# A fused attention, Fourier and MLP kernel: GpSimd's decay work waits for VectorE's progress, and decayed keys get two buffers

## What is computed

```python
for b in range(nb):                       # blocks of a sequence
    intra = einsum('bhic,bhjc->bhij', qb, kb) * Dmask     # scores, masked with the decay
    intra = einsum('bhij,bhjd->bhid', intra, vb)
    inter = einsum('bhid,bhde->bhie', qb * lam_pow, kv_state)   # decayed queries
    out[block] = intra + inter
    kb_dec = kb * rev_pow                                       # decayed keys
    kv_state = lam_block * kv_state + einsum('bhsd,bhse->bhde', kb_dec, vb)
# then, with x of 2 x 768 x 512:
u  = x + real(fft(fft(x, axis=seq), axis=hidden))
un = layernorm(u)
x2 = u + relu(un @ w_ch1) @ w_ch2                         # 512 -> 2048 -> 512
out = (sigmoid(causal_conv5(x2)) * (x2 @ w_val)) @ w_out
```

## Time and profile before

| | us |
|---|---|
| median of 3 runs | 451.03 |
| lowest and highest | 449.82 to 452.81 |
| the profiled execution | 451.31 |
| its span | 449.5 |

### The profile page before, as it was taken

The page is one execution under the profiler, slowest core; times in us unless marked ns, Lnnn a source line. Parts: engine busy times, 40 slices in busy tenths (PEclk is TensorE's granted clock), DMA queues, the critical chain, the costliest instruction groups (busy, mean ns, idle before and its releaser), DMA issues.

```text
span 449.5 us, 7168 instructions
## 1 busy us (share of the span) xinstructions
PE 434.8 (97%) x2934; PEld 415.0 (92%) x2934; DVE 264.5 (59%) x433; ACT 150.2 (33%) x284; POOL 146.4 (33%) x97
## 2 busy tenths in 40 slices
PE   9799869899999999999999999999999999999997
PEld 8688769789999999999999999999999999889985
DVE  2446897978356944454424327948557548999220
ACT  1145342274212331113342227353124233515221
POOL 1334461158422222523539223234224251500000
PEclk9899989999999999999999999999999999999999
DMA  6968720224022030202112212012112110001112
GB/s 202 382 211 273 206 79 2 65 59 158 2 93 94 0 95 1 93 1 94 55 41 95 54 41 93 29 66 95 34 61 93 32 63 2 1 1 70 71 47 93
DMA packets 13889, 36.52 MB, mean 81 GB/s; under 512 B 1561, under 2 KB 3105, under 8 KB 13857
## 3 DMA queue, kind: packets, MB, share of 16 engines
q1 hardware_dynamic: 13856, 36.07, 24.0%
HBM read 32.91 MB, written 3.15 MB: 80 GB/s over the span
## 4 chain that ended last, share of the span: by engine, by line
PE 85%; DVE 9%; DMA 2%; issue 2%; ACT 1%; SPq 1%; DVEq 0%
PE ps L532 10%; PE ps L534 10%; PE ps L555 10%; PE ps L533 10%; PE ps L554 10%; PE ps L553 10%; PE ps L644 2%; PE ps L643 2%; PE ps L642 2%; PE ps L621 2%; PE ps L622 2%; PE ps L623 2%; PE ps L406 2%; PE ps L489 2%; DMA chunks<-in_qkv 2%
## 5 line engine op out<-in xcount | busy, mean ns | idle before, releaser
L728 ACT ACTIVATE hh<-ps 128x384 fp32r<-128x384 f32 x64 | 31.5, 493 | 176.8 <-PE ps L534 176.8
L992 DVE SCALAR_TENSOR_TENSOR hl<-ps,hh 128x384 fp32r<-128x384 f32 x64 | 35.3, 556 | 87.0 <-ACT hh L728 87.0
L532 PE MATMUL ps<-cen_h,w1h_a 128*128 128x384 f32 x128 | 43.9, 343 | 0.5 <-DVE hl L992 0.5
L532 PE MATMUL ps<-cen_h,w1h_b 128*128 128x384 f32 x128 | 44.2, 345 | 0.0
L534 PE MATMUL ps<-cen_h,w1l_b 128*128 128x384 f32 x128 | 43.1, 337 | 0.0
L555 PE MATMUL ps<-hh,w2l_b 128*128 128x384 f32 x128 | 43.1, 337 | 0.0
L533 PE MATMUL ps<-cen_l,w1h_a 128*128 128x384 f32 x128 | 43.1, 337 | 0.0
L534 PE MATMUL ps<-cen_h,w1l_a 128*128 128x384 f32 x128 | 43.1, 337 | 0.0
L554 PE MATMUL ps<-hl,w2h_b 128*128 128x384 f32 x128 | 43.1, 337 | 0.0
L553 PE MATMUL ps<-hh,w2h_b 128*128 128x384 f32 x128 | 43.1, 337 | 0.0
L533 PE MATMUL ps<-cen_l,w1h_b 128*128 128x384 f32 x128 | 43.0, 336 | 0.0
(11 more groups left out here) (161 smaller groups left out, 1016.9 us busy)
## 6 DMA issues: line engine op xcount, KB each, us to landing
raw_a<-in_mlp SPq DMA_DIRECT2D x16, 512.0 KB, 4.7
raw_b<-in_mlp SPq DMA_DIRECT2D x16, 512.0 KB, 4.4
chunks<-in_qkv SPq DMA_DIRECT2D x12, 512.0 KB, 5.5
chunks<-in_qkv SPq DMA_DIRECT2D x22, 256.0 KB, 5.7
out<-out_sb SPq DMA_DIRECT2D x12, 256.0 KB, 2.0
raw_a<-in_val SPq DMA_DIRECT2D x2, 512.0 KB, 4.4
raw_b<-in_out SPq DMA_DIRECT2D x2, 512.0 KB, 4.4
seq_c<-const_seq SPq DMA_DIRECT2D x1, 768.0 KB, 6.0
```

Source lines behind the costliest of these rows:

```text
L532: mm(bank, wh_, xh, start=r == 0, stop=False)
L728: nc.scalar.activation(hh[:, slot, j], ps[j][:, 0:TB], ACT.Relu).then_inc(s_hh, 1)
L992: stt(hl[:, slot, j], ps[j][:, 0:TB], 0.0, hh[:, slot, j].bitcast(F32), ALU.max, ALU.subtract).then_inc(s_hl, 1)
```

## The change

GpSimd gets a wait at the head of each chunk from n = 6 on, on a count that VectorE raises (`turn_of`), and `kd` gets a second buffer, so that kd(n) waits for the state product two chunks back instead of the last. For n = 6 and 7 the wait is for the end of radix4(n - 2), for n = 8 for two_even, for n = 9 for chunk_pair(0, 2), for n = 10 for third_pair, and for n = 11 for add_pair(0, 1).

```diff
-            kd = sb_in(att, "kd", [P, H, Dh])
+            kd = sb_in(att, "kd", [P, 2, H, Dh])
...
-                        m = mm(ps[KV][par * Dh:(par + 1) * Dh, hp * Dh:(hp + 1) * Dh], kd[:, 2 * hp + par, :],
+                        m = mm(ps[KV][par * Dh:(par + 1) * Dh, hp * Dh:(hp + 1) * Dh], kd[:, kds(n) % 2, 2 * hp + par, :],
...
-                if kds(n) >= 2:
-                    pool.wait_ge(s_kv, kds(n) - 1)
-                tt(kd[:, :, :], kr[c], decay[:, :, 0:1].broadcast_to([P, H, Dh]), ALU.mult).then_inc(s_kd, 1)
+                if kds(n) >= 3:
+                    pool.wait_ge(s_kv, kds(n) - 2)
+                tt(kd[:, kds(n) % 2], kr[c], decay[:, :, 0:1].broadcast_to([P, H, Dh]), ALU.mult).then_inc(s_kd, 1)
...
+            def turn_of(n):
+                if n in (NC, NC + 1):
+                    pool.wait_ge(s_r4, R4 * (n - 1))
+                elif n == NC + 2:
+                    pool.wait_ge(s_r6, 6)
+                elif n == NC + 3:
+                    pool.wait_ge(s_r6, 10)
+                elif n == NC + 4:
+                    pool.wait_ge(s_r6, R6)
+                elif n == NC + 5:
+                    pool.wait_ge(s_u, added_u(0, 1))
+
             decay_keys(0)
             for n in range(1, N):
+                turn_of(n)
                 if n % NC < NC - 1:
                     decay_keys(n)
```

## The result

| | before | changed |
|---|---|---|
| median, us (runs) | 451.03 (6) | 446.87 (6) |
| lowest and highest | 449.82 to 452.81 | 445.40 to 448.07 |
| the profiled execution | 451.31 | 448.07 |
| its span | 449.5 | 446.3 |

The ratio of the two medians is 0.9908. Estimated from all the runs of both it is 0.9893, with a 95% interval of 0.9865 to 0.9921: between 0.8 and 1.35% faster. The forecast for the median was 447.1.

A forecast was written before the change was run, and what follows sets the result against it. VectorE and GpSimd were taken to block each other in SBUF, with TensorE waiting before a full MLP. The path, 69.16 - 65.3 = 3.9 us shorter, took 451.31 to 447.4, 447.1 for the median; range 445.6 to 449.0.

The forecast's parts named there:

- Chunk 7: kd(7) waits for radix4(5), so L898 takes 0.28 instead of 1.15: minus 0.87 us, in full on the path.
- L914 absorbed by mask(8)'s wait: In two_even, L914 waits 0.8 us for qd(7); VectorE's 1.12 us idle before mask(8) hides it, leaving 0.3.
- Chunk 8: kd(8) runs after two_even; L919's start to L920's end goes from 2.39 to 1.60 us: minus 0.79.
- Chunk 9: qd(9) still collides with L925, whose length goes from 1.16 to 1.42 us: plus 0.26.
- Chunk 10: kd(10), qd(10) and qd(11) leave the last three sums; L928 to L930 go from 4.89 to 2.04 us: minus 2.85.
- Behind it: After L930, radix4(6) waits for qd(10) and loses 0.8 us; seq_pair(0, 1) starts at 65.3 instead of 69.16.
- The front, zero: Early chunks: qd(3) delays radix4(1) but is hidden, and kd(4)'s keys land too late to collide; cost zero, bounds 0 and 0.8.
- The rule held against the change: A skill rule has the blocked engine start 0.25 us later in three collisions: gain an estimated 0.5 less, 3.4.
- queries slip through: Rival, chance 0.20: qd(10) doesn't go ahead of radix4(6), and qd(8), qd(9) collide less; gain 4.9, 446.1 us.
- the gates do little: Rival, chance 0.08: VectorE waits for TensorE's scores at every mask, only the first 0.87 us reaches the end; 450.2 us.
- The front collision: Rival, chance 0.17: kd(4)'s keys land before 25.8 us, so kd(4) meets radix4(1); gain 3.1, 447.9 us.
- The clock falls: Rival, chance 0.05: TensorE's clock falls in the gap from 63.7 to 65.3 us and stays low to 78; net 2 slower, 453.

The follow-up runs named there:

- e2: The changed kernel without its second key buffer, so the gates alone; 446.42 us, ratio 0.9915 to before.
- e3: The kernel with one key buffer and all gates, cut to only the gates of chunks 10 and 11; 447.90 us, ratio 0.9942 to before.
- e6: The changed kernel with one gate more, qd(10) waiting for radix4(6); 446.47 us, ratio 0.9892 to before.
- e5: The changed kernel with qd(8), qd(9) and qd(10) computed for only 8 of 128 tokens; 443.94 us, ratio 0.984 to before.
- e10: The changed kernel with one gate more, hidden_sum(0, 2) on GpSimd waiting for radix4(8); 445.84 us, ratio 0.9877 to before.
- e8: The changed kernel with the first MLP weights loaded after chunk 4 instead of chunk 3, so chunk 4's keys land earlier; 447.78 us, ratio 0.9919 to before.
- e1: The changed kernel without its gates, so two key buffers alone; 451.03 us, ratio 1.0011 to before.
- e7: The changed kernel with batch 0's decayed keys waiting for the last state product, as before the change; 446.76 us, ratio 0.9904 to before.
- e9: The kernel before with 13 unused products on TensorE in the wait before seq_pair(0, 0), to keep the clock up; 449.62 us, ratio 0.9978 to before.

## Why the prediction was right

The forecast was 447.1 us, with 3.9 us of gain on the path; measured were 446.87 us, and 4.27 to seq_pair(0, 1). The forecast gave 0.69 to a change within 1% and 0.27 to a faster one; with 0.8 to 1.35% the result lies on the border of the two, or just beyond. Times of the changed profile are given less 1.21 us here, on the common point.

- *Chunk 7*, minus 0.87: L898 0.28, and TensorE's wait fell by 0.86.
- *L914 absorbed by mask(8)'s wait*: 0.3 was to be left of 1.12; 0.43 was. mask(8) at 50.25, forecast 50.29.
- *Chunk 8*, minus 0.79: L919's start to L920's end 1.47 instead of 1.60; before 2.39. e2 shows that the second buffer is what buys it.
- *Chunk 9*, L925 1.42: 1.38.
- *Chunk 10*, minus 2.85: exactly; L930 ended at 60.32, forecast 60.50. e3 shows this gate, with that of chunk 11, at 2.7 of 4.3, its cost in radix4(6) included.
- *Behind it*: radix4(6) lost 0.69, forecast 0.8; e6 takes it away. seq_pair(0, 1) started 4.27 earlier, forecast 3.9. I put the 0.37 down to small sizes: I charged 0.1 for each gate's handover, which took 0.08, and let an operation start at the recorded end of the one before, where it starts 0.08 before that. Behind seq_pair(0, 1), where I had the same chain, another 0.23 was gained to the MLP (4.50 in all); hidden_sum(0, 1) met radix4(7)'s L892 for 0.2 (0.3 forecast).
- *The front, zero*: it held, in this profile by a margin of nothing. All engines in order of time around radix4(1) of the changed kernel:

```profile
26.92 0.28 DVE L898 TENSOR_TENSOR zin<-esum 128x128 f32<-128x128 f32 x1
...
27.23 1.06 POOL L1156 TENSOR_TENSOR kd<-chunks,decay 128x512 f32<-128x512 f32 x1 [1.05 <-DMA chunks<-in_qkv]
...
27.50 0.71 PE L464 MATMUL ps<-hid_c,zin 128*128 128x128 f32 x4
```

radix4(1) ends at 27.20, 0.3 before TensorE needs it, and kd(4), whose keys came late, starts 0.03 behind. On the common point these are 25.99 (25.98 forecast) and 26.02 (26.2). In the three other profiles with this front and the same loads kd(4) starts later behind radix4(1): 0.3 us in e5, 1.7 in e6, 1.4 in e10. e8 shows the price when the keys don't come late. In how many executions of the changed kernel that happens stays open.

- *The rule held against the change* from the Trainium skill, SBUF — State Buffer, section "A bandwidth-pool intuition that's wrong", was an estimated 3.4. The measured 4.27 speaks for the rows: L914, L919 and L925 ended 0.54 to 0.55 after the qd that held them and are 0.68 long, so it began before the blocker's recorded end, here as before.
- *The rivals*: "queries slip through" is what e5 builds, and it was not the case; "the gates do little" fell with L930. "The front collision" is what e8 builds; it cost 0.7. "The clock falls" was half right: behind a gap of 1.6 us it did fall in two profiles of relatives of this kernel (e3 and e10), and cost 1.6 us, since it came back after 3.4 us and not at 78. I had ruled it nearly out from one gap of 1.65 that left the clock alone. The changed kernel's one profile doesn't show it behind this gap, and it can't have happened in the two runs with a mean clock of 1.00. Where the low stretch of its other three runs lay is not known.

What the forecast didn't have is the race of hidden_sum(0, 2). Its profile of before happened to show the long form, as did the changed kernel's, so the error canceled: luck, since five of the eleven profiles without the gate have the short form. Its effect between two profiles (1.14 us) is a quarter of the whole change.

## What to carry to other kernels

Where GpSimd's work on SBUF runs beside VectorE operations with two inputs in SBUF, count lengths per operation, not only idle time: the loss hides inside the busy time. Let GpSimd wait for the VectorE step behind which VectorE reads PSUM, and give its tiles enough buffers to follow; here a buffer without a gate only moved the collisions (e1). A second GpSimd operation behind the first needs a place of its own: the masks here hold one of 1.06 us, not 2.2.

## What was not expected of the hardware

- The order in which the two engines get their turn isn't fixed by who was there first. GpSimd's L298, asked for 0.16 us into L892, went in front of L895 (2.04 us) in the changed kernel and behind L895, L897 and L898 in e7 (L298 2.68 instead of 1.93).
- The granted clock fell to 0.50 after waits of 0.52 and 1.60 us in e3, and stayed at 1.00 after waits of 0.73 and 1.61 us in e2, at the same places of the list. A low stretch lasted 3.4 us each time. It cost 1.5 us between scores(2) and radix4(3) and 1.6 behind seq_pair(0, 1), but only 0.5 to 0.8 behind the hole of the kernel before (e9), where TensorE mostly waited for VectorE.
